# A masked product run twice in the first batch, three reorderings, and the last output tile in two column halves

## The reference

```python
# 1: attention, 8 heads of 64, window of 128 keys, a bias linear in the distance
scores = scale * q @ k.T - slope[h] * |i - j|      # only 0 <= i - j < 128
x = softmax(scores) @ v                             # (B, S, 512)
# 2: spatial gating unit
h = relu(x @ w_in); u, v = h[..., :512], h[..., 512:]
v_s = einsum('ts,bsd->btd', w_spatial, layernorm(v)) + b_spatial
g = (u * v_s) @ w_out
# 3: mixture of 4 attention experts (causal), the 2 best by the gate
w = softmax over the two best of (g @ w_gate)
out = sum over e of w_e * softmax(causal(q_e @ k_e.T / 8)) @ v_e @ wo[e]
```

## Time and profile before

| | us |
|---|---|
| three runs | 496.26, 496.90, 498.81 |
| median | 496.9 |
| profiled execution, its own time | 496.05 |
| its span in the trace | 494.2 |
| PE busy | 474.0 (96%) |
| DVE, ACT, POOL busy | 320.9, 271.7, 213.6 |

### The profile page before, as it was taken

One profiled execution on the slowest core, in us unless ns is written; L12 is line 12 of the kernel. 1 busy time (PEld: TensorE's weight loads), 2 busy tenths in 40 slices (PEclk: granted clock), 3 DMA queues, 4 the chain that ended last, 5 costly groups with the idle time before them and its releaser, 6 DMA issues.

```text
span 494.2 us, 10632 instructions
## 1 busy us (share of the span) xinstructions
PE 474.0 (96%) x3794; PEld 404.1 (82%) x3794; DVE 320.9 (65%) x1247; ACT 271.7 (55%) x822; POOL 213.6 (43%) x378
## 2 busy tenths in 40 slices
PE   8689989999999999999999999999999999999996
PEld 5457989899776789999776779999876779999874
DVE  6886875257778855437778865436777975335783
ACT  5667563246676744235666654335666663335663
POOL 4494628222344526742253525760443442461431
PEclk9999999999999999999999999999999999999999
DMA  7927520003201073002311063001311000000111
GB/s 235 320 55 217 201 86 0 1 2 76 91 22 44 2 197 91 1 1 48 109 34 44 1 184 106 0 2 40 95 44 56 1 1 2 0 2 8 42 43 54
DMA packets 33512, 31.64 MB, mean 64 GB/s; under 512 B 6002, under 2 KB 24434, under 8 KB 33460
## 3 DMA queue, kind: packets, MB, share of 16 engines
q1 hardware_dynamic: 33460, 30.97, 20.6%
HBM read 23.88 MB, written 4.72 MB: 58 GB/s over the span
## 4 chain that ended last, share of the span: by engine, by line
PE 73%; DVE 14%; ACT 7%; issue 3%; POOL 2%; DVEq 0%; POOLq 0%
PE bank L1385 16%; PE bank L1387 15%; PE bank L1386 15%; PE bank L1372 6%; PE bank L1450 6%; ACT p L825 4%; PE bank L1412 3%; DVE ring L936 3%; PE bank L1614 3%; PE bank L1629 2%; PE bank L1651 2%; DVE p L1170 2%; PE bank L1391 2%; PE bank L1392 1%; POOL ring L542 1%
## 5 line engine op out<-in xcount | busy, mean ns | idle before, releaser
L542 POOL TENSOR_SCALAR ring<-ring,r 128x128 f32<-128x128 f32 x144 | 62.4, 447 | 80.1 <-DVE r L956 79.8
L628 POOL TENSOR_SCALAR p<-p,r,wgt 128x128 f32<-128x128 f32 (+3 forms) x64 | 38.6, 616 | 92.9 <-DVE wgt_last L1217 49.9
L656 ACT ACTIVATE ring<-ring,neg 128x128 f32<-128x128 f32 x144 | 56.7, 396 | 23.9 <-DVE ring L947 19.4
L825 ACT ACTIVATE p<-p,neg 128x128 f32<-128x128 f32 (+4 forms) x72 | 41.7, 580 | 31.9 <-DVE neg L1170 31.9
L936 DVE CUSTOM_DVE_ANT_0 ring<-bank,bias 128x256 f32<-128x256 f32 (+1 forms) x128 | 43.7, 385 | 6.1 <-PE bank L1372 5.6
L1372 PE MATMUL bank<-k,q 64*128 64x256 f32 (+2 forms) x320 | 39.0, 372 | 2.8 <-DVE neg L936 2.8
L592 POOL TENSOR_TENSOR g_lo<-uT,g_hi 128x288 fp32r<-128x288 f32 x32 | 26.8, 862 | 32.1 <-ACT g_hi L791 32.1
L1385 PE MATMUL bank<-g_hi,w_c_hi 128*128 128x288 f32 x128 | 38.3, 299 | 2.1 <-DVE k_lo L1273 2.1
L1385 PE MATMUL bank<-w_spatial_hi,vn_hi 128*128 128x288 f32 x128 | 37.9, 296 | 2.3 <-DVE uT L1149 2.3
L1385 PE MATMUL bank<-x_hi,w_in_hi 128*128 128x288 f32 x128 | 38.2, 298 | 0.0
L1387 PE MATMUL bank<-x_hi,w_in_lo 128*128 128x288 f32 x128 | 37.7, 294 | 0.0
(11 more groups left out here) (193 smaller groups left out, 1447.7 us busy)
## 6 DMA issues: line engine op xcount, KB each, us to landing
v_in<-v SPq DMA_DIRECT2D x16, 256.0 KB, 3.9
out<-o_sb SPq DMA_DIRECT2D x16, 256.0 KB, 2.0
q<-qT SPq DMA_DIRECT2D x15, 256.0 KB, 4.5
k<-kT SPq DMA_DIRECT2D x15, 256.0 KB, 4.8
v_minus_v_of_tile_above<-v SPq DMA_DIRECT2D x9, 256.0 KB, 3.9
w_in_raw<-w_in SPq DMA_DIRECT2D x4, 512.0 KB, 5.7
w_cat_raw<-wcat SPq DMA_DIRECT2D x1, 1544.0 KB, 7.1
w_spatial_raw<-wsT SPq DMA_DIRECT2D x1, 1152.0 KB, 8.6
```

The costliest lines, as they stand in the source:

```text
L542: last = nc.gpsimd.tensor_scalar(p, p, r1[:, i % 2, h:h + 1], 0.0, ALU.mult, ALU.add)
L628: nc.gpsimd.tensor_scalar(p, p, r3[:, i % 2, e:e + 1], by, ALU.mult, ALU.mult).then_inc(s3_sd, 1)
L656: nc.scalar.activation(x, x, ACT.Exp, bias=neg1[:, u % SLOTS1:u % SLOTS1 + 1], scale=-1.0, accum_out=sum1[:, i % 2, h:h + 1]).then_inc(s1_ ...
L825: nc.scalar.activation(p, p, ACT.Exp, bias=neg3[:, w % 4:w % 4 + 1], scale=-1.0, accum_out=sum3[:, i % 2, es[0]:es[0] + 1]).then_inc(s3_ex, 1)
```

## The change

In the first batch the difference of v is no longer made. ACT writes `v_step[:, t] = -v_in[t]` for t = 0 to 3 (`negate_v`, in the steps m = 1, 3, 5, 7), and PE multiplies the masked weights twice, with v of the own tile and with the negated v of the tile above. The memset of `masks` moves from POOL to a copy on ACT near the start of the program. In the later batches POOL's differences stay as they are.

The low parts of `w_cat` move on DVE from in front of the gates to behind gate 3: two of them go with each low part of `w_outT` ahead of the gates 4 to 7. On ACT `high_qk(4)` moves ahead of `exp3(0)` and `exp3(1)`; DVE's order there stays. `high_z(0)` moves from step 1, where it stood ahead of `copy_pt3(1)`, into step 0 between `exp3(8)` and `exp3(9)`. `out_product` does the products with the high part of z first, and for the second half of the two last tiles waits for the low part only then. The last output tile is made in two column halves in banks 6 and 5; ACT copies one, DVE the other, and SP stores each by itself.

```diff
--- before.py
+++ after.py
@@ -455,6 +459,11 @@
                         load_v(b + 1, t)
                 for i, qb in enumerate(ORDER3):
                     sp.wait_ge(s3_o, NT * b + i + 1)
+                    if not more and i == NT - 1:
+                        sp.dma_start(out[b, tok(qb), 0:HD], o_sb[:, 0, 0:HD]).then_inc(s_out[0], 16)
+                        sp.wait_ge(s3_o2, 1)
+                        sp.dma_start(out[b, tok(qb), HD:DM], o_sb[:, 0, HD:DM]).then_inc(s_out_last, 16)
+                        continue
                     sp.dma_start(out[b, tok(qb), :], o_sb[0:rows(qb), i % 2, :]).then_inc(s_out[i % 2], 16)
 
             row(0, True, True)
...
@@ -499,7 +509,7 @@
 
                     link(nc.gpsimd.affine_select(out=causal[:], in_=causal[:], compare_op=ALU.is_ge, fill=MASKED, base=0,
                                                  pattern=[[-1, P]], channel_multiplier=1))
-                    link(nc.gpsimd.memset(masks[:], 0.0))
+                    pool.wait_ge(s_mz, 1)
                     link(nc.gpsimd.tensor_copy(masks[:, 512 + LAST + 512 - P:512 + LAST + 512], causal[:]))
                     for odd in range(2):
                         link(nc.gpsimd.tensor_copy(masks[D * odd:D * odd + D, 512:512 + LAST], causal[0:LAST, 0:LAST]))
@@ -518,12 +528,6 @@
             nc.gpsimd.affine_select(out=diag[:], in_=diag[:], compare_op=ALU.is_ge, fill=0.0, base=0,
                                     pattern=[[1, P]], channel_multiplier=-1).then_inc(s_diag, 1)
 
-            def first_v_step(t):
-                pool.wait_ge(s_v_in[t - 1], 16)
-                pool.wait_ge(s_v_in[t], 16)
-                r = rows(t)
-                nc.gpsimd.tensor_tensor(v_step[0:r, t - 1], v_in[0:r, t], v_in[0:r, t - 1], ALU.subtract).then_inc(s_vd, 1)
-
             def v_steps(b):
 
                 pool.wait_ge(s_vs_in, 16 * NT * b)
...
@@ -567,8 +571,6 @@
                     for g in (2 * m + 3, 2 * m + 4):
                         if g < NG1:
                             scale1(b, g)
-                        if first and g < NG1 and g % 4 == 1:
-                            first_v_step(g // 4)
                     if first and m in TABLES_AT:
                         tables(TABLES_AT.index(m), 2 * m + 5)
                 pool.wait_ge(s1_xl, NT * (b + 1))
@@ -657,8 +659,10 @@
                                          accum_out=sum1[:, i % 2, h:h + 1]).then_inc(s1_ex, 1)
 
             act.wait_ge(s_warm, 1)
-            nc.scalar.copy(v_step[LAST:P, NT - 2], pt_hi[LAST:P, 0, 0:D].bitcast(F32).unsqueeze(1).to_broadcast([P - LAST, H, D])
+            nc.scalar.copy(v_in[LAST:P, NT - 1], pt_hi[LAST:P, 0, 0:D].bitcast(F32).unsqueeze(1).to_broadcast([P - LAST, H, D])
                            ).then_inc(s_vz0, 1)
+            nc.scalar.copy(masks[:].rearrange("p (a c) -> p a c", c=LAST),
+                           pt_hi[:, 0, 0:LAST].bitcast(F32).unsqueeze(1).to_broadcast([P, 1024 // LAST + 1, LAST])).then_inc(s_mz, 1)
             exp1(0, 0)
             exp1(0, 1)
             exp1(0, 2)
@@ -701,6 +705,10 @@
                 def high_x(i):
                     act.wait_ge(s1_pv, NG1 * b + END1[i] + 1)
                     nc.scalar.copy(x_hi[:, :, tok(ORDER1[i])], xt_of(i)).then_inc(s1_xh, 1)
+
+                def negate_v(t):
+                    act.wait_ge(s_v_in[t], 16)
+                    nc.scalar.activation(v_step[:, t], v_in[:, t], ACT.Copy, scale=-1.0).then_inc(s_vneg, 1)
 
                 def relu_v(i):
                     act.wait_ge(s1_vm, NT * b + i + 1)
@@ -751,6 +759,8 @@
                             exp1(b, 2 * m + 4)
                     if m == ND1 - 3:
                         exp1(b, NG1 - 1)
+                    if first and m % 2 and m < ND1 - 1:
+                        negate_v(m // 2)
                     for half, at in W_IN_AT.items():
                         for k in range(KT):
                             if first and at[k] == m:
@@ -873,9 +883,9 @@
                 copy_v3(1)
                 copy_v3(NT - 1)
                 exp_logits(0)
+                high_qk(4)
                 exp3(0)
                 exp3(1)
-                high_qk(4)
                 exp3(2)
                 exp3(3)
                 high_qk(5)
@@ -888,7 +898,7 @@
                 copy_v3(2)
                 copy_v3(3)
                 for m in range(ND3):
-                    for i in range(NT - 2):
+                    for i in range(1, NT - 2):
                         if m == DEND3[i] + 1:
                             high_z(i)
                     for i in (NT - 2, NT - 1):
@@ -899,6 +909,8 @@
                         if m == DEND3[i] + 2:
                             copy_out(b, i)
                     for w in units3(m):
+                        if w == 2 * E + 1:
+                            high_z(0)
                         exp3(w)
                     if more and m >= ND3 - 3:
                         exp1(b + 1, m - (ND3 - 3))
@@ -911,7 +923,9 @@
                 if more:
                     exp1(b + 1, 3)
                 else:
-                    copy_out(b, NT - 1)
+                    act.wait_ge(s3_om, NT * B)
+                    act.wait_ge(s_out[0], OUTS[0] * b + 16 * ((NT - 1) // 2))
+                    nc.scalar.copy(o_sb[:, 0, 0:HD], bank[:, 6, 0:HD]).then_inc(s3_o, 1)
 
             row(0, True, True)
             for b in range(1, B - 1):
@@ -1128,20 +1142,18 @@
                 if not first:
                     dve.wait_ge(s2_um, 8 * (b + 1))
                     nc.vector.memset(v3[LAST:P, AT3[NT - 1]], 0.0).then_inc(s_vz3, 1)
-                if first:
-                    for d in range(KT):
-                        dve.wait_ge(s_fsh, d + 1)
-                        nc.vector.tensor_tensor(wcat_lo[:, d, 0:CUT], wcat_raw[:, d, 0:CUT], wcat_qk_hi[:, d, :].bitcast(F32),
-                                                ALU.subtract).then_inc(s_fsl, 1)
-                    for d in range(KT):
-                        dve.wait_ge(s_fsh, KT + d + 1)
-                        nc.vector.tensor_tensor(wcat_lo[:, d, CUT:CW], wcat_raw[:, d, CUT:CW], wcat_v_hi[:, d, :].bitcast(F32),
-                                                ALU.subtract).then_inc(s_fsl, 1)
+                def low_w_cat(d, c0, c1, high, n):
+                    dve.wait_ge(s_fsh, n)
+                    nc.vector.tensor_tensor(wcat_lo[:, d, c0:c1], wcat_raw[:, d, c0:c1], high[:, d, :].bitcast(F32), ALU.subtract
+                                            ).then_inc(s_fsl, 1)
+
                 for i in range(8):
                     a, dt = divmod(i, 4)
                     c = slice(HALF * a, HALF * a + HALF)
                     if first and i >= 4:
                         d = i - 4
+                        low_w_cat(d, 0, CUT, wcat_qk_hi, d + 1)
+                        low_w_cat(d, CUT, CW, wcat_v_hi, KT + d + 1)
                         dve.wait_ge(s_fsh, 2 * KT + d + 1)
                         nc.vector.tensor_tensor(woT_lo[:, d, :], woT_raw[:, d, :], woT_hi[:, d, :].bitcast(F32),
                                                 ALU.subtract).then_inc(s_fsl, 1)
@@ -1338,6 +1350,10 @@
                 if more:
                     bias1(b + 1, 5)
                     join1(b + 1, 5)
+                else:
+                    dve.wait_ge(s3_om, NT * B + 1)
+                    dve.wait_ge(s_out[0], OUTS[0] * b + 16 * ((NT - 1) // 2))
+                    nc.vector.tensor_copy(o_sb[:, 0, HD:DM], bank[:, 5, 0:HD]).then_inc(s3_o2, 1)
 
             row(0, True, True)
             for b in range(1, B - 1):
@@ -1416,17 +1432,50 @@
                 r = rows(ORDER3[i])
                 if i == 0 and b == 0:
                     pe.wait_ge(s_wlo, 2 * KT + NT + 2)
-                for k in ks:
-                    if k == ks[0] or i >= NT - 2:
-                        pe.wait_ge(s3_zl, z_count(b, i, k))
+                to = bank[:, 6 + i % 2, :]
+                for part in [ks] if i < NT - 2 else [(k,) for k in ks]:
                     if r < P:
-                        last = stacked(bank[:, 6 + i % 2, :], zt[:, i % 2, k, P - r:P + r], wo_hi[:, k, :], wo_lo[:, k, :],
-                                       k == 0, k == 1)
+                        pe.wait_ge(s3_zl, z_count(b, i, 0))
+                        for k in part:
+                            last = stacked(to, zt[:, i % 2, k, P - r:P + r], wo_hi[:, k, :], wo_lo[:, k, :], k == 0, k == 1)
                         continue
-                    last = three(bank[:, 6 + i % 2, :], zt[:, i % 2, k, 0:P], zt[:, i % 2, k, P:2 * P],
-                                 wo_hi[:, k, :], wo_lo[:, k, :], k == 0, k == 1)
+                    if part[0] == 0:
+                        pe.wait_ge(s3_zl, z_count(b, i, 0))
+                    else:
+                        pe.wait_ge(s3_zh, z_count(b, i, 1))
+                    for k in part:
+                        nc.tensor.matmul(to, zt[:, i % 2, k, 0:P], wo_hi[:, k, :], start=(k == 0), stop=False)
```

(39 more changed lines are left out.)

7 lines of the change are left out of this document (6 added, 1 removed).

## The result

| | before | after |
|---|---|---|
| median of 20 runs each | 496.85 us (495.23 to 498.81) | 498.78 us (497.40 to 499.87) |
| profiled execution, span | 496.05, 494.2 us | 499.87, 498.0 us |
| ratio, 95% interval | 1 | 1.0036 (1.0024 to 1.0047) |

What follows compares the result with a forecast made beforehand. PE, busy 96% of the span, was taken as the bound; 0.4 + 0.0 + 1.7 - 2.4 - 0.3 = -0.6 us gave 495.45 from 496.05, or 496.3 against the median; 8-in-10 range 493.8 to 499.1 us.

Steps and rivals of the forecast that it cites:

- A: First batch, stage 1: doubled product and zeroing on ACT; added products cost 2.1 us, earlier start gains 1.7; +0.4 us.
- B: First batch, low parts of w_cat behind the gates: the gates' 2.3 us wait moves to `fold`; sum 0.0 us.
- C: `high_qk(4)` ahead of the exps: k's low part, behind DVE's reciprocal, starts 0.43 us later each batch; +1.7 us.
- D: `high_z(0)` in step 0: PE's wait for z's low part goes, with gains further on; -2.4 us in four batches.
- E: Output products and the end: high products first give 0, the last copy in halves ends earlier; -0.3 us.
- 0.4 us before each of the four rounds: DVE's low-part rounds before `fold`: DVE loses 0.4 us to a POOL operation ahead of each round.
- the next two places: Behind the output product, where PE is handed work late: moving `high_z(0)` gains about 0.2 us more there.
- Rival (1): First batch, stage 1: PE is the bound from step 2 on, added products count; +2.1 us, 499.0 us; 20%.
- Rival (2): Low parts ahead of `fold`: DVE's rounds aren't held up, `fold` starts at 80.4; -2.4 us, 494.5 us; 14%.
- The bound of +0.8 for B: Upper limit for moving w_cat's low parts behind the gates: one more POOL operation let in, +0.8 us.

## Why the prediction was wrong, point by point

| part | forecast | by the traces | by the run with it undone |
|---|---|---|---|
| A | +0.4 | -0.1 | 0.0 |
| B | 0.0 | +3.8 | +3.1 |
| C | +1.7 | +1.3 | +1.2 |
| D | -2.4 | -2.3 | -2.4 |
| E | -0.3 | -0.45 | 0.0 |
| sum | -0.6 | +2.2 | +1.9 |

The last column is 1.0036 less the ratio with the part undone, times 496.85; each has an uncertainty of about 1 us, so that it orders B and D and does no more for A, C and E.

**B is the step that failed, twice.** The place of the new wait was right (`fold`, on the low parts), and so was the mechanism. Its size was not: a wait of about 2.5 us was forecast, 4.5 came. Of the missing 2 us, the "0.4 us before each of the four rounds" was the mis-sized term. I let POOL in once a round, because in the earlier trace rows two subtractions in a row had kept POOL out. In the first round POOL had four low parts of g waiting and got in between DVE's operations each time: 1.7 us lost there, then 0.9, 0.6 and 0.6, where 0.4 each was forecast. So seven collisions cost 3.8 us where four were put at 1.6. The rounds took 11.2 us, not the 9.2 of the sum. The price of one disturbed subtraction stood in the earlier trace rows (1.30 us, 0.62 more than alone); what I had no row for was how many of them would be disturbed, and I took the lower count. The Trainium skill, page "SBUF — State Buffer", section "Who interferes with whom", by which two such operations exclude each other for a whole instruction and the order of issue decides who blocks, agrees with the lengthened subtractions here (by 0.51 to 0.62 us in six of seven), and with the run in which POOL was silent, where none was lengthened.

The second half of B, the clock, stood nowhere in the prediction. I took a wait of PE to be worth its length. Yet before, too, its 2.3 us cost more than their length in many executions, 1.0 us over all of them. What the change added is then the difference of the two losses, not the whole one, which is why the traces (one of before without any loss) can give B 3.8 us and the medians 3.1. I had noticed that the profiled execution lies 0.85 us under the median and added that as a constant; this loss is the likely reason, with the scatter of the start as another that wasn't taken apart.

**A** came out near its forecast with the working half right. DVE's chain was 0.64 us earlier at its low part of w_in, the wait for `ring` went, and PE was 1.72 us earlier there (1.7 forecast). The products added behind it cost 1.64 us net, not 2.1, which is the whole difference from +0.4 to -0.1. What I missed is that the memset was enough: with it on ACT, POOL's differences leave PE 0.9 us of waits, and the double product that frees them costs 1.0 us more than it gives.

**C**'s mechanism was right (k_lo behind the reciprocal); the term was 0.43 us a batch and measured 0.32; of the difference 0.09 is that the low part starts 0.29 us behind `den`, where 0.38 was taken. **D** was right in mechanism and size: -0.6 a batch forecast, -0.58 by the distance between batches, with zt's low part 1.02 us earlier (0.9 forecast). That 0.2 of it would come at the next two places was wrong, and the total is in part luck: all of it comes at the output product. **E** was right by the trace (0.32 from the halves, 0.13 from the rest) and is out of reach of the medians.

**The rivals.** Rival (1) gave 499.0 us, next to the 498.78 measured, and was still wrong: by its mechanism A would cost 1.8 to 2.0 and D give 1.3, while A costs nothing and D gives 2.4. Rival (2), B pays 1.8 us if nothing holds DVE's rounds up, is what the run with POOL held back shows: `fold` starts 1.81 us earlier than before. The bound of +0.8 for B, "one more POOL operation let in", was too tight: the first round alone let in two more, and nothing in the bounds stood for what comes after a wait.

## What to carry to other kernels

When work is moved on an engine, count which operations of the engine that holds it up (POOL for DVE here) are already queued at that time, and charge one collision for each of them, up to one for each operation moved, not one for each group. Price a wait of the matmul engine at its length plus what the clock loses behind it, and read each execution's granted clock, and where it was lower, before taking one profiled execution as the base: filling 2.3 us of idle time with products that nobody reads gained 1.0 to 1.4 us here. When two edits remove the same wait, try each alone; the cheaper one may leave the other only its cost.
